# Scores of two of three tiles made three rounds ahead of their selection, in a ring of five rounds

## The chip, the cores and the metric
The kernel runs on 1 core of one Trainium2 chip. The metric is the device time of one execution in microseconds (us); the median over several runs is taken.

## The reference
Three stages in fp32, one behind the other:

```python
# attention: batch 4, 8 heads, 576 tokens, head size 64
scores = scale * np.matmul(q, k.transpose(0, 1, 3, 2))
kth = np.partition(scores, -32, axis=-1)[..., -32:-32 + 1]
scores = np.where(scores >= kth, scores, -1e9)
attn = softmax(scores)                      # exp(s - max) / (sum + 1e-9)
x = matmul(attn, v)                         # -> 2304 x 512
# maxout: d_model 512, d_ff 768
x = np.maximum(np.maximum(x @ w1, x @ w2), x @ w3) @ w_out
# experts: 8, top 1 by x @ w_gate + bias of the row's modality, 512 -> 1024 -> 512
out[mask] = gate_w[mask, None] * (np.maximum(x[mask] @ w1[e], 0.0) @ w2[e])
```

## The kernel before, in words
Attention works in 48 rounds. A round is one block of 192 queries for a pair of heads, 384 rows of scores over 576 keys, held as three tiles of 128 rows: tile 0 and 1 are the first 128 queries of the two heads, tile 2 the remaining 64 of both. Tiles 0 and 1 are folded, which halves what the top-32 selection must search: instead of the scores of each head, TensorE makes the scores against the second half of the keys (index 0, for both heads) and the scores against the difference of the two halves of the keys (index 1, for both heads). From these GpSimd's `fold` makes `upper` and `lower` (the larger and the smaller of each pair of scores) and the scores of the first half. Index 2 is tile 2 in full, against all keys. So only (r, 1) needs `k_diff`, the key differences that GpSimd makes; (r, 0) and (r, 2) go through the same PSUM tile `s_ps`, and (r, 1) through `t_ps` (`d_ps` in the code), which the transposes use too. ScalarE copies (r, 0) and (r, 2) from PSUM to the ring `scores` and (r, 1) to `rise` and `fall` (two instructions).

Each engine runs its own list in order, the rounds being software-pipelined. In round r:

- TensorE (`one_round`, order from `round_items(r)`): the items are Q (a score product), V (the value products of round r-3), H (transposes of the probabilities of round r-2, in five steps) and M (groups of the maxout stage, rounds 6 to 53, and before it W, a product of weights, in rounds 2 to 5). With `AHEAD = 2` the Q items are those of round r+2. The order is Q0, Q1, V, M, H, H, Q2, H, H, M, H, M. The scores of rounds 0 and 1 are made ahead of round 0.
- ScalarE: the copies of these in the same order, and between them the steps of the masked exponential: for round r the scalars, `below` of tiles 0 and 1; for round r-1 `below` of tile 2 (behind Q1) and the three exponentials (behind Q1 to ahead of the copy of Q2).
- VectorE: the selection (MAX8 and MATCH_REPLACE8) of round r, 13 us, and the sums and inverses of round r-1.
- GpSimd, round r: `leave_out(r-1)` (L811, three subtractions of `below`), `add_ways`, `key_differences(r+3)` (L753), `fold(r+2)` (L764, L765, L767), `divide(r-1)` (L819), and up to round 5 `weight_difference(r+2)` (L833).
- SyncE: its queue of loads. In round r it waits for the values' buffer and issues `load_v(r-1)`, then `load_qk(r+4)` (keys L642, queries L643, the rest of the queries in two parts L648) once the tiles of round r+2 are scored, since keys and queries have two slots. Behind the loads of rounds 0 and 1 stand the loads of the weights of the maxout stage, of the biases and of `modality` (one element to a piece).

Maxout takes three groups in a round (`PARTS`), its first group is the first item M of round 6 and waits for all eight weight differences. Up to round 45 there are Q items; then the order is V, M, H, H, M, H, H, M, H. Behind the attention the last rounds finish the maxout stage, and then the experts run.

`scores` has `RING = AHEAD + 2` rounds of three tiles of 576 columns. Counting semaphores carry the order: `scores_ready` (TensorE made a tile) and `scores_copied` (ScalarE copied it) are compared with `scored(r, i)`, the tile's place in the order.

```python
def scored(r, i):
    return r * GROUP + score_order(r).index(i) + 1
```

Of the kernel before, what the change touches and what calls it, by code (L numbers as in the profile page):

```python
# [27 lines left out]
ROUNDS = BLOCKS * RPB  # L28
# [4 lines left out]
GROUP = 3  # L33
REST = BLK - P
AHEAD = 2
LAG = 2
PROB_BUFS = 2
assert PROB_BUFS >= LAG
RING = AHEAD + 2
HALF = SEQ // 2  # L40
FULL = SEQ // P
KB = FULL + 1
# [64 lines left out]
def wait_apart(eng, passed, sem, value):  # L107


    eng.wait_ge(sem, value)  # L110
    eng.sem_inc(passed, 1)
# [65 lines left out]
def score_order(r):  # L177


    return (2, 0, 1) if r == 0 else (0, 1, 2)  # L180


def scored(r, i):


    return r * GROUP + score_order(r).index(i) + 1


def in_range(r):

    return 0 <= r < ROUNDS


def finished_units(r):

    return [(m, g[1]) for m, g in maxout_groups(r) if g[0] == "A" and g[2] == WAYS - 1]
# [5 lines left out]
def round_items(r):  # L202

    ahead, middle, behind = ([("M",) + g for g in groups] for groups in maxout_thirds(r))
    q = [("Q", i) for i in range(GROUP)] if in_range(r + AHEAD) else [None] * GROUP
    h = [("H", c) for c in range(KB)] if in_range(r - LAG) else [None] * KB
    v = ("V",) if in_range(r - LAG - 1) else None
    if in_range(r + AHEAD):  # L210
        items = [q[0], q[1], v] + ahead + h[:2] + [q[2]] + h[2:4] + middle + h[4:] + behind
    else:
        items = [v] + ahead + h[:2] + middle + h[2:4] + behind + h[4:]
    return [item for item in items if item is not None]
# [216 lines left out]
def program(nc, qT, kT, v, w_in, w3T, w_out, w_gate, modality, bias, e_w1, e_w2, shared, x2_dram, list_dram, out):  # L431

    with ExitStack() as ctx:
# [44 lines left out]
        with ExitStack() as held:  # L478
# [10 lines left out]
            v_sb = hb("v_sb", [P, 2, KB, 2 * HEAD])  # L489
            scores = hb("scores", [P, RING, GROUP, SEQ])  # L490
            rise = hb("rise", [P, FOLDED, HALF])
# [53 lines left out]
        passed = sem("passed")  # L545
# [10 lines left out]
        scores_ready = sem("scores_ready")  # L556
        scores_copied = sem("scores_copied")
# [76 lines left out]
        def _(sp):  # L634
            def load_qk(r):

                slot = r % 2
                if r >= 2:

                    sp.wait_ge(scores_ready, (r - 1) * GROUP)  # L640
                k_of = r // (BPB * RPB) * PPB + r % PPB
                sp.dma_start(k_sb[:, slot, :], kT[k_of, :, :]).then_inc(qk_in[slot], 16)  # L642
                sp.dma_start(q_sb[:, slot, :], qT[r, :, 0:P]).then_inc(qk_in[slot], 16)  # L643
                if r < 2:

                    sp.wait_ge(rest_pads_ready, 1)
                for h in range(2):
                    sp.dma_start(q_rest[h * HEAD:(h + 1) * HEAD, slot, h * HEAD:(h + 1) * HEAD],  # L648
                                 qT[r, h * HEAD:(h + 1) * HEAD, P:BLK]).then_inc(qk_in[slot], 16)
# [90 lines left out]
        def _(pool):  # L740
# [15 lines left out]
            def fold(r):  # L756

                slot, ring = r % FOLD_BUFS, r % RING
                wait_apart(pool, passed, scores_copied, scored(r, 1))
# [168 lines left out]
        def _(act):  # L928
# [30 lines left out]
            def copy_scores(r, i):  # L959

                act.wait_ge(scores_ready, scored(r, i))
                part = (d_ps if i == 1 else s_ps)[:, :, 0:HALF]
                if i == 0:
                    nc.scalar.copy(scores[:, r % RING, 0:FOLDED, HALF:SEQ], part).then_inc(scores_copied, 1)
                elif i == 1:
                    if r > 0:

                        act.wait_ge(fold_step, r * 3)
                    nc.scalar.activation(rise[:, :, :], part, ACT.Relu)
                    nc.scalar.activation(fall[:, :, :], part, ACT.Relu, scale=-1.0).then_inc(scores_copied, 1)  # L970
                else:
                    nc.scalar.copy(scores[:, r % RING, i, :].rearrange("p (h n) -> p h n", h=2), part)\
                      .then_inc(scores_copied, 1)
# [52 lines left out]
            def one_round(r):  # L1026
                steps = []
                if in_range(r - 1):
                    steps += [(NEXT_ROUND[name], step) for name, step in zip(STEPS, softmax_steps(r - 1))
                              if name in NEXT_ROUND]  # L1030
                if in_range(r):
                    steps += [(THIS_ROUND[name], step) for name, step in zip(STEPS, softmax_steps(r))
                              if name in THIS_ROUND]
                for m, u in finished_units(r - 1) if r <= LOAD_AT else LAST_UNITS if r == RECTIFY_LAST else []:
                    steps.append((RECTIFY_AT if in_range(r - 1) else -1, lambda m=m, u=u: rectify(m, u)))
                if r == RECTIFY_LAST:
                    for n in range(PIECES // 2):
                        steps.append((-1, lambda n=n: high_piece(0, n)))
                steps.sort(key=lambda step: step[0])
                ran = 0  # L1040
                for item, at in places_in_round(r):

                    while ran < len(steps) and steps[ran][0] < at:
                        steps[ran][1]()
                        ran += 1
                    if item[0] == "H":
                        copy_probsT(r - LAG, item[1])
                    elif item[0] == "Q":
                        copy_scores(r + AHEAD, item[1])
                    elif item[0] == "V":  # L1050
                        copy_out(r - LAG - 1)
                    elif item[2][0] != "Y":
                        copy_moe(*item[1:])
                        if r >= RECTIFY_LAST and item[2] in TURN_AT:
                            for n in TURN_AT[item[2]]:
                                x_high_part(0, n)
                for _, step in steps[ran:]:
                    step()
# [25 lines left out]
            act.wait_ge(sum_pads_ready, 1)  # L1084
            nc.scalar.activation(warm[:, :], sums[:, 0, 0, 1:2], ACT.Exp)
            act.wait_ge(pads_ready, 2)
            for r in range(AHEAD):
                for i in score_order(r):
                    copy_scores(r, i)
            for r in range(LAST_ROUND):  # L1090
                one_round(r)
                if r == COUNT_AT:
# [244 lines left out]
        def _(pe):  # L1337
            def score_tile(r, i):

                slot = r % 2  # L1340
                if i == score_order(r)[0]:
                    pe.wait_ge(qk_in[slot], (r // 2 + 1) * QK_LOADS)
                if i == 1:
                    wait_apart(pe, passed, k_diff_ready, r + 1)
                    turned = (r - AHEAD - LAG) * KB
                    if turned > 0:

                        wait_apart(pe, passed, probsT_copied, turned)
                    elif r > 0:

                        wait_apart(pe, passed, scores_copied, scored(r - 1, 1))
                else:
                    other = scored(r, 2) if (r, i) == (0, 0) else scored(r, 0) if (r, i) != (0, 2) and i == 2 \
                        else scored(r - 1, 2) if r > 1 else scored(0, 0)
                    if (r, i) != (0, 2):

                        wait_apart(pe, passed, scores_copied, other)
                if i < 2:

                    keys = k_sb[:, slot, HALF:SEQ] if i == 0 else k_diff[:, slot, :]  # L1360
                    for h in range(2):
                        ins = nc.tensor.matmul((s_ps if i == 0 else d_ps)[:, h, 0:HALF], q_sb[h * HEAD:(h + 1) * HEAD, slot, :],  # L1362
                                               keys[h * HEAD:(h + 1) * HEAD, :], start=True, stop=True)
                else:

                    for half in range(2):
                        ins = nc.tensor.matmul(s_ps[:, half, 0:HALF], q_rest[:, slot, :],  # L1367
                                               k_sb[:, slot, half * HALF:(half + 1) * HALF], start=True, stop=True)
                ins.then_inc(scores_ready, 1)
# [94 lines left out]
            def one_round(r):  # L1464
                for item in round_items(r):
                    if item[0] == "H":
                        transpose_keys(r - LAG, item[1])
                    elif item[0] == "Q":
                        score_tile(r + AHEAD, item[1])
                    elif item[0] == "V":  # L1470
                        weigh_values(r - LAG - 1)
                    else:
                        moe_group(*item[1:])
# [36 lines left out]
                                               start=(f == 0 and i == 0), stop=(f == FB2 - 1 and i == 2))  # L1510
                ins.then_inc(y_ready, 1)

            for r in range(AHEAD):
                for i in score_order(r):
                    score_tile(r, i)
            for r in range(RECTIFY_LAST):
                one_round(r)
                if r == COUNT_AT:
# [78 lines left out]
```

## Time and profile before

| | us |
|---|---|
| median of 3 runs | 943.24 (943.15 to 943.54) |
| the profiled execution | 943.44 |
| its span, first to last instruction | 941.8 |
| TensorE matmul busy | 897.8 |
| VectorE busy | 720.3 |
| GpSimd busy | 660.1 |
| ScalarE busy | 567.7 |

The profile is of one execution. "Span" is from its first to its last instruction, and what lies around it (1.6 us) is not in the trace. PE is TensorE's matmul, PEld its weight load, DVE is VectorE, ACT is ScalarE, POOL is GpSimd, SP is SyncE. A busy share is an average over stages; the windows give it by stretch.

### The profile page before, as it was taken

The page shows a single profiled execution, that of the slowest core. Times are in us where ns is not written, and L with a number is a line of the kernel's source. Part 1 is how long each engine was busy: PE and PEld are TensorE (multiplying, and loading weights), DVE is VectorE, ACT ScalarE, POOL GpSimd, SP SyncE. Part 2 cuts the span into 40 slices and gives each one's busy share as a digit, 9 for nine tenths or more (in the row PEclk, how much of TensorE's full clock was granted, in tenths as well). Part 3 has the DMA queues.
Part 4 walks back from the last instruction along what each step waited for, and adds up shares of the span by engine and source line. Part 5 has one row for each costly group of instructions (what it writes and reads, how often), then busy time and mean ns, then how long its engine had stood idle before and what let it go on. Part 6 is the DMA issues. An engine that isn't in the chain of part 4 may idle for free.

```text
span 941.8 us, 17739 instructions
## 1 busy us (share of the span) xinstructions
PE 897.8 (95%) x5132; PEld 693.6 (74%) x5133; DVE 720.3 (76%) x2191; ACT 567.7 (60%) x1274; POOL 660.1 (70%) x624
## 2 busy tenths in 40 slices
PE   6688999999999999999999999999999999999997
PEld 2344868668695787759686786858685898998996
DVE  6999999999999999999999999998803721251211
ACT  3577678688877787678786787776533322341221
POOL 7999898988988799878988889885562412231221
PEclk9999999999999999999999999999999999999999
DMA  7721112221211222122121212111052161116110
GB/s 243 220 57 49 53 50 71 82 88 53 66 52 43 70 59 71 43 70 60 46 68 47 82 49 66 47 37 37 14 164 88 40 208 58 54 32 236 45 56 33
DMA packets 69271, 70.84 MB, mean 75 GB/s; under 512 B 15456, under 2 KB 50560, under 8 KB 69184
## 3 DMA queue, kind: packets, MB, share of 16 engines
q1 hardware_dynamic: 65264, 59.44, 20.9%
q0 software_dynamic: 3920, 10.40, 3.5%
q8 instruction: 36, 0.59, 0.2%
q14 instruction: 51, 0.42, 0.1%
HBM read 59.05 MB, written 10.76 MB: 74 GB/s over the span
## 4 chain that ended last, share of the span: by engine, by line
PE 87%; ACT 4%; POOL 3%; issue 3%; DVE 1%; DMA 1%; SPq 1%; POOLq 0%; ACTq 0%; DVEq 0%
PE m_ps L1427 20%; PE m_ps L1509 11%; PE m_ps L1453 9%; PE o_ps L1400 8%; PE s_ps L1492 8%; PE t_ps L1384 7%; PE m_ps L1441 7%; PE s_ps L1367 4%; PE s_ps L1362 3%; PE t_ps L1362 3%; PE o_ps L1492 3%; PE m_ps L1460 2%; POOL scores L811 1%; PE m_ps L1446 1%; DMA q_rest<-queries_t 1%
## 5 line engine op out<-in xcount | busy, mean ns | idle before, releaser
L811 POOL TENSOR_TENSOR scores<-scores,below 128x576 f32<-128x576 f32 x144 | 201.1, 1414 | 65.3 <-ACT below L945 64.7
L1427 PE MATMUL m_ps<-xT,w_sb 128*128 128x192 f32 x1152 | 201.9, 330 | 2.0 <-POOL w_sb L833 2.0
L1427 PEld LDWEIGHTS m_ps<-xT,w_sb 128*128 128x128 f32 x1152 | 187.3, 192 | 5.7 <-issue 5.7
L1155 DVE MAX8 top<-upper 128x8 f32<-128x288 f32 x384 | 159.3, 448 | 0.3 <-issue 0.3
L980 ACT COPY probsT<-t_ps 128x384 f32<-128x384 f32 x240 | 106.6, 491 | 38.2 <-PE t_ps L1384 38.1
L1157 DVE MATCH_REPLACE8 upper<-top,upper 128x288 f32<-128x288 f32 x288 | 125.3, 443 | 0.2 <-issue 0.2
L953 ACT ACTIVATE probs<-scores,shift 128x576 f32<-128x576 f32 x144 | 111.7, 782 | 16.3 <-issue 11.0
L1384 PEld LDWEIGHTS t_ps<-ident,probs 128*128 128x128 f32 x720 | 86.2, 141 | 44.1 <-issue 19.5
L819 POOL TENSOR_SCALAR probs<-probs,inverse 128x576 f32<-128x576 f32 x144 | 105.3, 752 | 16.5 <-DVE inverse L1145 16.5
L1384 PE MATMUL t_ps<-ident,probs 128*128 128x128 f32 x720 | 103.6, 275 | 12.8 <-ACT probsT L980 12.8
L945 ACT ACTIVATE below<-scores,steep_kth 128x576 f32<-128x576 f32 x144 | 109.4, 777 | 2.2
L1155 DVE MAX8 top<-work 128x8 f32<-128x576 f32 x144 | 107.2, 744 | 0.4
L889 POOL DMA_INDIRECT out_rows<-y_sb,info x18 | 17.9, 996 | 108.2 <-ACT y_sb L1081 107.5
L1400 PE MATMUL o_ps<-probsT,v_sb 128*64 128x192 f32 x960 | 88.9, 332 | 2.9 <-issue 2.9
L1453 PE MATMUL m_ps<-wo_sb,stage 128*128 128x512 f32 x192 | 86.3, 598 | 0.0
L1400 PEld LDWEIGHTS o_ps<-probsT,v_sb 128*64 128x64 f32 x960 | 65.7, 137 | 27.4 <-issue 20.8
L1155 DVE MAX8 top<-lower 128x8 f32<-128x288 f32 x192 | 77.2, 445 | 0.0
L1244 DVE SCALAR_TENSOR_TENSOR hTl<-s_ps,hTh 128x384 fp32r<-128x384 f32 x36 | 19.8, 556 | 68.1 <-ACT hTh L1073 68.1
L1157 DVE MATCH_REPLACE8 work<-top,work 128x576 f32<-128x576 f32 x96 | 71.3, 743 | 0.0
L1008 ACT ACTIVATE stage<-m_ps 128x384 f32<-128x384 f32 x72 | 35.1, 488 | 59.3 <-PE m_ps L1427 59.3
L764 POOL TENSOR_TENSOR upper<-scores,rise 128x576 f32<-128x576 f32 x48 | 68.0, 1417 | 0.9 <-ACT fall L970 0.9
L765 POOL TENSOR_TENSOR lower<-scores,fall 128x576 f32<-128x576 f32 x48 | 68.0, 1416 | 0.0
(208 smaller groups left out, 1780.1 us busy)
## 6 DMA issues: line engine op xcount, KB each, us to landing
k_sb<-keys_t SPq DMA_DIRECT2D x48, 288.0 KB, 2.6
v_sb<-values SPq DMA_DIRECT2D x48, 256.0 KB, 2.7
raw<-e_w SPq DMA_DIRECT2D x12, 1024.0 KB, 5.1
maxout_rows<-x_rows SPq DMA_DIRECT2D x18, 256.0 KB, 2.2
q_sb<-queries_t SPq DMA_DIRECT2D x48, 64.0 KB, 2.5
w_sb<-w SPq DMA_DIRECT2D x2, 1536.0 KB, 8.5
q_rest<-queries_t SPq DMA_DIRECT2D x96, 16.0 KB, 2.3
v_sb<-values SPq DMA_DIRECT2D x48, 32.0 KB, 2.6
```

The lines of the kernel that those rows point to most:

```text
L811: nc.gpsimd.tensor_tensor(scores[:, r % RING, i, :], scores[:, r % RING, i, :], below[:, i, :], ALU.subtract).then_inc(masked_ready, 1)
L819: nc.gpsimd.tensor_scalar(part, part, inverse[:, r % 2, i:i + 1], 0.0, ALU.mult, ALU.add)\
L945: nc.scalar.activation(below[:, i, :], scores[:, r % RING, i, :], ACT.Relu, bias=steep_kth[:, top_slot, i:i + 1], scale=-STEEP).then_inc(b ...
L953: nc.scalar.activation(probs[:, r % PROB_BUFS, i, 0:SEQ], scores[:, r % RING, i, :], ACT.Exp, bias=shift[:, top_slot, i:i + 1], scale=SCAL ...
L980: nc.scalar.copy(probsT[:, :, c, :], d_ps[:, c % 2, 0:2 * BLK].rearrange("p (h q) -> p h q", h=2))\
L1155: nc.vector.max(best, src).then_inc(topk_step, 1)
L1157: nc.vector.match_replace(dst, best, src, LOWEST).then_inc(topk_step, 1)
L1384: ins = nc.tensor.transpose(d_ps[:, c % 2, at:at + P], probs[:, r % PROB_BUFS, i, c * P:(c + 1) * P], ident[:, :])
L1400: ins = nc.tensor.matmul(o_ps[h * HEAD:(h + 1) * HEAD, 0:BLK], v_sb[:, slot, c, h * HEAD:(h + 1) * HEAD], probsT[:, h, c, :], start=(c == ...
L1427: ins = nc.tensor.matmul(dst[:, a * BLK:(a + 1) * BLK], w_sb[:, w, c, (first + a) * P:(first + a + 1) * P], xT[:, m % 2, c, b % SPAN * BLK ...
L1453: ins = nc.tensor.matmul(dst[:, :], hT[:, m % 2, j, i * P:(i + 1) * P], wo_sb[:, j, :], start=False, stop=(j == FB - 1))
L1509: ins = nc.tensor.matmul(y_ps[n % 2][:, :], h[:, f, n * P:(n + 1) * P], w[:, f, :], start=(f == 0 and i == 0), stop=(f == FB2 - 1 and i == 2))
```

## The change
`(r, 0)` and `(r, 2)` are made three rounds ahead, in round r-3; `(r, 1)` stays two rounds ahead. The ring has five rounds instead of four. The prologue makes two tiles more, `(2, 0)` and `(2, 2)`. The place of a tile in the order is now looked up in a table, and the load of keys and queries waits for the last tile of the round whose slot it takes.

```diff
-RING = AHEAD + 2
+WHOLE_AHEAD = AHEAD + 1
+RING = WHOLE_AHEAD + 2
...
+def ahead_of(i):
+    return AHEAD if i == 1 else WHOLE_AHEAD
+
+FIRST_SCORES = [(r, i) for r in range(AHEAD) for i in score_order(r)] \
+    + [(r, i) for r in range(AHEAD, WHOLE_AHEAD) for i in (0, 2)]
+SCORES = FIRST_SCORES + [(r + ahead_of(i), i) for r in range(ROUNDS) for i in range(GROUP) if r + ahead_of(i) < ROUNDS]
+SCORED = {tile: n + 1 for n, tile in enumerate(SCORES)}
+DIRECT = [tile for tile in SCORES if tile[1] != 1]
...
 def scored(r, i):
-    return r * GROUP + score_order(r).index(i) + 1
+    return SCORED[r, i]
+
+def all_scored(r):
+    return max(scored(r, i) for i in range(GROUP))
...
-    q = [("Q", i) for i in range(GROUP)] if in_range(r + AHEAD) else [None] * GROUP
+    q = [("Q", i) if in_range(r + ahead_of(i)) else None for i in range(GROUP)]
...
 # load_qk(r), SyncE
-                    sp.wait_ge(scores_ready, (r - 1) * GROUP)
+                    sp.wait_ge(scores_ready, all_scored(r - 2))
...
 # ScalarE, one_round
-                        copy_scores(r + AHEAD, item[1])
+                        copy_scores(r + ahead_of(item[1]), item[1])
...
 # ScalarE, ahead of round 0
-            for r in range(AHEAD):
-                for i in score_order(r):
-                    copy_scores(r, i)
+            for r, i in FIRST_SCORES:
+                copy_scores(r, i)
...
 # TensorE, score_tile(r, i), i = 0 or 2
-                    other = scored(r, 2) if (r, i) == (0, 0) else scored(r, 0) if (r, i) != (0, 2) and i == 2 \
-                        else scored(r - 1, 2) if r > 1 else scored(0, 0)
-                    if (r, i) != (0, 2):
-                        wait_apart(pe, passed, scores_copied, other)
+                    n = DIRECT.index((r, i))
+                    if n > 0:
+                        wait_apart(pe, passed, scores_copied, scored(*DIRECT[n - 1]))
...
 # TensorE, one_round
-                        score_tile(r + AHEAD, item[1])
+                        score_tile(r + ahead_of(item[1]), item[1])
...
 # TensorE, ahead of round 0
-            for r in range(AHEAD):
-                for i in score_order(r):
-                    score_tile(r, i)
+            for r, i in FIRST_SCORES:
+                score_tile(r, i)
```

## Rows read from the trace of the kernel before

**Rows 1.** The page, part 1: busy us, share of the span, instructions.
```profile
PE 897.8 (95%) x5132; PEld 693.6 (74%) x5133; DVE 720.3 (76%) x2191; ACT 567.7 (60%) x1274; POOL 660.1 (70%) x624
```

**Rows 2.** Windows: length, then PE, PEld, DVE, ACT, POOL busy, PEclk, DMA, GB/s.
```profile
26.00:70.00 44.00, 32.67 (x140) 17.92 (x137) 42.71 (x136) 29.62 (x64) 44.00 (x38) 0.96 0.41 124
...
88.00:95.80 7.80, 4.67 (x37) 2.91 (x37) 7.62 (x26) 7.16 (x16) 7.80 (x8) 1.00 0.25 67
...
330.00:440.00 110.00, 108.61 (x671) 81.86 (x670) 106.83 (x339) 83.41 (x197) 96.37 (x87) 1.00 0.21 60
```

**Rows 3.** Timeline at the first maxout group: start, us, engine, line, operation, idle before.
```profile
93.91 1.81 POOL L833 TENSOR_TENSOR w_sb<-w_sb,stage 128x768 f32<-128x768 f32 x1
...
95.86 4.52 PE L1427 MATMUL m_ps<-xT,w_sb 128*128 128x192 f32 x16 [2.01 <-POOL w_sb L833]
```

**Rows 4.** Timeline of a steady round: its score load and the next round's first product.
```profile
385.18 0.33 SPq L642 DMA_DIRECT2D k_sb<-keys_t  x1
...
386.12 1.11 SPq L648 DMA_DIRECT2D q_rest<-queries_t  x2
...
391.27 0.76 PE L1362 MATMUL s_ps<-k_sb,q_sb 64*128 64x288 f32 x4
```

**Rows 5.** The chain that ended last, at the start: start, us, what.
```profile
24.79 1.33 PE s_ps L1362 x4
26.13 0.97 PE t_ps L1362 x4
...
29.81 2.12 DMA q_rest<-queries_t
```

**Rows 6.** Timeline of all engines from 19 to 36 us.
```profile
19.02 0.64 ACT L964 COPY scores<-s_ps 128x576 f32<-128x576 f32 x1 [1.53 <-PE s_ps L1362]
...
20.35 2.29 PE L1367 MATMUL s_ps<-k_sb,q_rest 128*128 128x288 f32 x4
...
22.67 6.11 SPq L642 DMA_DIRECT2D k_sb<-keys_t  x1
...
25.34 1.42 POOL L764 TENSOR_TENSOR upper<-scores,rise 128x576 f32<-128x576 f32 x1
...
29.30 1.11 SPq L648 DMA_DIRECT2D q_rest<-queries_t  x2
...
29.58 0.65 ACT L969 ACTIVATE rise<-t_ps 128x576 f32<-128x576 f32 x1 [2.68 <-POOL scores L767]
...
30.66 0.78 ACT L945 ACTIVATE below<-scores,steep_kth 128x576 f32<-128x576 f32 x1
...
31.21 4.12 POOL L811 TENSOR_TENSOR scores<-scores,below 128x576 f32<-128x576 f32 x3
...
35.28 0.80 POOL L753 TENSOR_TENSOR k_diff<-k_sb 128x288 f32<-128x288 f32 x1
```

**Rows 7.** DMA issues from 14 to 40 us: count, KB each, us to landing.
```profile
mod<-modality SPq DMA_DIRECT2D x1, 18.0 KB, 9.0
```

**Rows 8.** The chain that ended last, round 45: (47, 0), then (47, 2).
```profile
624.08 0.69 PE s_ps L1362 x4
...
631.56 0.97 PE s_ps L1367 x4
```

**Rows 9.** Timeline: pairs of probability copies and the transposes behind them, two places.
```profile
88.28 0.86 ACT L980 COPY probsT<-t_ps 128x384 f32<-128x384 f32 x2
...
88.81 0.93 PE L1384 MATMUL t_ps<-ident,probs 128*128 128x128 f32 x6 [0.89 <-ACT probsT L980]
...
631.42 0.87 ACT L980 COPY probsT<-t_ps 128x384 f32<-128x384 f32 x2
...
632.37 0.82 PE L1384 MATMUL t_ps<-ident,probs 128*128 128x128 f32 x6
```

**Rows 10.** Timeline of VectorE in round 46.
```profile
649.85 0.16 DVE L1140 TENSOR_REDUCE full_sum<-sums 128x3 f32<-128x6 f32 x1 [2.13 <-ACT probs L953]
```

**Rows 11.** TensorE's waits from 90 to 640 us: us in total, times, longest.
```profile
PE t_ps L1384 <- ACT probsT L980: 6.5, 7, 1.1
```

More of the change, by code:

```diff
@@ L180, in score_order @@
     return (2, 0, 1) if r == 0 else (0, 1, 2)
+def ahead_of(i):
[4 more added lines that the diff above has]
+SCORED = {tile: n + 1 for n, tile in enumerate(SCORES)}
+assert len(SCORED) == len(SCORES) == ROUNDS * GROUP
+DIRECT = [tile for tile in SCORES if tile[1] != 1]
 def scored(r, i):
-    return r * GROUP + score_order(r).index(i) + 1
+    return SCORED[r, i]
+def all_scored(r):
+    return max(scored(r, i) for i in range(GROUP))
 def in_range(r):
```

## Prediction
> **How I read it.** The windows come first, to see which engine has no slack in which stretch; then what ends the wait at the seam between two stretches; then the timeline around the moved tiles, at the start and at the end. A tile is written (round, index): the change moves (r, 0) and (r, 2), not (r, 1).
>
> **What bounds the kernel now.** TensorE is busy for 897.8 of 941.8 us, GpSimd for 660.1 [rows 1]. By stretch it is two machines. From 26 to 70 us GpSimd is busy for all of its 44.00 us, TensorE for 32.67; from 88 to 95.8 GpSimd for 7.80 of 7.80, TensorE for 4.67. From 330 to 440 us TensorE is busy for 108.61 of 110, GpSimd for 96.37 [rows 2]. The seam is at 95.86: the first maxout group has kept TensorE idle for 2.01 us, until GpSimd's last weight difference, begun at 93.91, was done [rows 3]. Before the seam a wait of GpSimd costs its full length, since it has no idle time to make it up from; behind the seam only TensorE's work and idle time count.
>
> **What stays.** Every product, copy and fold is still made once. In rounds 3 to 44 the items stand in the same places, and each product into the shared score bank still waits for the copy before it. The ring grows with the distance, so its reuse adds no wait. Steady rounds should keep their length if keys and queries come in time. These have to be there a round earlier: tile (r+4, 0) opens round r+1, no longer r+2. Take one steady round: its score load goes out from 385.18 to 386.12 + 1.11 = 387.23; 2.12 us later, at 389.4, it has landed, and the next round opens at 391.27 [rows 4, 5]. Even sent as late as now it is in time, and it may go earlier, since it waits for (r+2, 1) and no longer for (r+2, 2). SyncE's other loads of the round are in front of it as before. Cost: nothing, under the cover of these 1.9 us and more; without it a round loses what is missing.
>
> **The start, where two tiles are added.** The prologue gets (2, 0) and (2, 2), which were round 0's; round 0 then makes (3, 0), (2, 1), (3, 2), and round 1 opens with (4, 0). TensorE has room for all of it. But (2, 1) and (3, 1) stand behind more than before, and GpSimd waits for their copies.
> Step 1. (2, 0) is copied at 19.02 for 0.64 us, as now. Then (2, 2), 2.29 long at this clock [rows 6], runs from 19.8 to 22.1; its copy ends near 22.8; (3, 0) starts then and (2, 1) ends 1.33 + 0.97 = 2.30 later [rows 5], at 25.1. Its two copies are over 1.2 us on (from 29.58 to just behind 30.66 in the round shown), at 26.4. The fold of round 2 starts at 25.34 now: it is 1.1 us late. A weight difference of 1.81 and two of the three subtractions (L811, 4.12 for three) are queued behind it; the third is reached at about 35.1, where it now starts at about 33.9 [rows 3, 6].
> Step 2. This third subtraction needs ScalarE's third `below` of round 0, which stands behind the copies of (3, 1). On TensorE (3, 1) stands behind (4, 0) after the change, and (4, 0) needs the load of round 4. SyncE begins that load at 22.67 and is held in it for 6.11 us, its last part goes out at 29.30, and the chain has it landed at 29.81 + 2.12 = 31.93 [rows 5, 6]. After the change SyncE comes to it at 25.1, when (2, 1) is scored, which is inside the hold. I take the hold to have a fixed end, because the load of the modality, of 18 KB in tiny pieces and issued just before, takes 9.0 us to land [rows 7], about as long as the hold lasts. So 31.93 stays; the same load sent later can't well land earlier.
> Step 3. (4, 0) starts at 31.97, (3, 1) ends 2.30 later at 34.3, its first copy starts at 34.4, `below` 1.08 after that (29.58 to 30.66 now) at 35.45, and ends 0.78 later at 36.25. The third subtraction starts about 0.15 behind it and takes 1.4: it ends at 37.8. The key difference behind it starts at 35.28 now [rows 6]. That is 2.5 us lost, and the 1.1 of step 1 are inside them. VectorE's sum for round 0 needs the last exponential, which stands behind the same subtraction, so VectorE is late by the same and no more.
> Step 4. Does anything swallow it? Behind it on GpSimd are fold 3, a division, and in order everything up to the weight difference of rows 3, with no idle time between, so the seam moves from 95.86 to 98.4. Is more added? (5, 0) waits for the copy of (4, 2), which stands behind the last exponential: 37.8 + 0.8 + 0.7 = 39.4. (4, 1) ends 2.3 later near 41.8, and its copy can't begin before fold 3 ends at 37.8 + 0.8 + 4.2 = 42.8. Nothing is added.
>
> The price of the hold can be doubted from a page. The Trainium skill (DMA: Bandwidth & Descriptors, section "Anatomy of one DMA — SWDGE (gpsimd) path") calls descriptor generation a small part of a transfer's fixed cost, of which many can be emitted before it shows; it speaks of another issuing path than SyncE's. The row of 6.11 us says otherwise for this load; by the page alone it would land before 29 us after the change too, only step 1 would be lost, and the sum would be 943.3. I keep the row.
>
> **The end, where two tiles are gone.** Round 45 has only (47, 1) left. On the chain there (47, 0) has 0.69 us and (47, 2) 0.97 [rows 8]. Without the first, the value products start right behind (47, 1), and 0.69 is gained. The second covers a copy as well. The transposes behind it need the pair of copies that begins at 631.42. Where a pair begun at 88.28 had no cover, the next six transposes started at 88.81 and ended at 89.74, 1.46 behind the copies' start; here that makes 632.88, against 632.37 + 0.82 = 633.19 now [rows 9]. So 0.3 of the 0.97 comes through. Sum 1.0; bounds nothing (both only covered) and 1.66 (neither did). VectorE doesn't take it back: in the next round it waits for ScalarE for 2.13 us [rows 10]. All behind is released by TensorE and moves along.
>
> **Sum.** +2.5 - 1.0 = +1.5 us. The profiled execution took 943.44 with a span of 941.8 and would take 944.9; it lies 0.2 over the median, so on 943.24 it makes 944.7. Bounds of the start: 1.1 if the load is never waited for, 5.0 if the hold keeps its length. The small steps may be off by 0.6 together, so the likeliest case alone spans 944.0 to 945.3.
>
> **Rivals.**
> A. The hold is a duration and not an end. SyncE is free at 25.1 + 6.1 = 31.2, the load lands at 34.4, 2.5 later, and the start costs 5.0: 943.24 + 5.0 - 1.0 = 947.2, slower. For it: there is only this one hold to judge by. Against: the slow load in front of it. It decides once the load lands 0.4 us later than now, as each us over 31.93 goes straight to the seam and 945.13 is the bound below. Chance 0.15.
> B. The load is earlier, and only step 1 is lost: 943.3. It needs a landing before 29.3, which a later issue can hardly give. Chance 0.09.
> C. GpSimd's delay is swallowed before the seam and only the end counts: 942.2. Against: 7.80 busy of 7.80. Chance 0.07.
> D. The larger distance frees the steady rounds: the waits of the transposes for ScalarE's copies, 7 of them with 6.5 us in all between 90 and 640 us [rows 11], go away: 943.24 + 1.5 - 6.5 = 938.2. Against: the score copy in front of it keeps its place. Chance 0.04.
> E. In steady rounds the score load comes late after all; a quarter of a us in each of 40 rounds is 10 us, 955. Against: rows 4. Chance 0.03.
> The forecast as worked out has 0.62.
>
> **Numbers.** A measurement of this kernel tells a change of about 0.2% from none, that is 1.9 us: same is 941.35 to 945.13. Slower: A, E and, as 944.7 lies near the bound, 0.12 of the forecast's 0.62, together 0.30. Faster: D and a little of C, 0.05. Same: 0.65. The range leaves out C, D, E and the outer parts of A and B, in all under 0.2: 943.0 to 947.3.
>
> **What would show it.** In the profile after: the hold of the `k_sb` load ending near 28.8 again; a GpSimd wait of about 1.1 us before the fold of round 2 and of about 1.3 before the third L811 of round 0; (4, 0) at 32.0; the first maxout group near 98.4, with some 2 us idle before it; still 6.5 us in waits for copies in the steady rounds; round 45 shorter by about 1.0. I am wrong if the hold ends past 29, if GpSimd shows idle time between 40 and 95 us, or if steady rounds change their length.

## The result and the profile after
The changed kernel took 944.13 us (median of 20 runs, 942.65 to 946.22), the kernel before 941.97 in the same comparison (20 runs, 941.6 to 943.69). The ratio is 1.0017, with a 95% interval of 1.0011 to 1.0023: 1.6 us more, on 943.24 some 944.8 (the two medians lie 2.2 us apart, at the upper end of the interval). Forecast were 944.7 and 0.16% more. The size is right, but the profile shows that two terms of the sum were too large and almost offset each other. The 943.24 of three runs, on which the forecast was built, lies in the upper of two groups of the kernel before: of its 20 runs 13 took 941.6 to 942.17 and 7 took 943.15 to 943.69.

The timeline of the changed kernel at the start and at the seam (line numbers are its own: L662 is the load of keys, L784 the fold, L831 the subtraction, L1380 and L1445 the score product and the maxout group):
```profile
25.12 1.85 SPq L662 DMA_DIRECT2D k_sb<-keys_t  x1
...
26.50 1.41 POOL L784 TENSOR_TENSOR upper<-scores,rise 128x576 f32<-128x576 f32 x1 [1.20 <-ACT fall L990]
...
30.56 1.33 PE L1380 MATMUL s_ps<-k_sb,q_sb 64*128 64x288 f32 x4 [3.45 <-DMA q_rest<-queries_t]
...
32.35 4.15 POOL L831 TENSOR_TENSOR scores<-scores,below 128x576 f32<-128x576 f32 x3
...
33.96 0.78 ACT L965 ACTIVATE below<-scores,steep_kth 128x576 f32<-128x576 f32 x1
...
36.44 0.81 POOL L773 TENSOR_TENSOR k_diff<-k_sb 128x288 f32<-128x288 f32 x1
...
97.02 2.84 PE L1445 MATMUL m_ps<-xT,w_sb 128*128 128x192 f32 x16 [2.00 <-POOL w_sb L853]
```
They answer to [rows 6] and [rows 3]. The fold of round 2 starts at 26.50 after a wait of 1.20 us, where 1.1 was expected. But SyncE's hold (the time for which it is kept in one issue, here that of the keys of round 4) ends at 26.97, not at 28.78; (4, 0) starts at 30.56, the third `below` ends at 34.74, and GpSimd, which comes to the third subtraction only at about 35.1, finds it ready. The key difference is at 36.44 against 35.28, the first maxout group at 97.02 against 95.86: 1.16 us, and none of the second wait. TensorE idles 2.00 us ahead of the seam as before.

The waits of TensorE from 90 to 640 us (total, times, longest) and a window of the steady rounds, from one wait for a copy to another, first after the change and then before it:
```profile
PE t_ps L1402 <- ACT probsT L1000: 7.8, 9, 1.1
...
PE t_ps L1380 <- ACT probsT L1000: 0.7, 1, 0.7
```
```profile
126.40:580.50 454.10, 447.33 (x2733) 333.17 (x2733) 441.65 (x1402) 346.29 (x812) 400.44 (x361) 1.00 0.22 63
...
126.90:580.80 453.90, 447.20 (x2733) 333.28 (x2733) 441.33 (x1401) 346.41 (x812) 400.49 (x361) 1.00 0.21 62
```
The steady rounds kept their length within 0.2 us: 454.10 against 453.90, and the bounds are rounded. From the wait at 144.01 to the one at 580.80 it is 436.79 us before the change; after it, from 143.69 to 580.55, it is 436.86. The waits for copies are 7.8 us in 9 where [rows 11] had 6.5 in 7; one of the nine, 0.90 at 89.98, was moved into the window by the delay ([rows 9] show it at 88.81), and one of 0.40 in round 45 is new. The other seven are those of [rows 11]. The second row, 0.7 us, is new. The chain shows where it stands:
```profile
623.49 0.34 PE t_ps L1402 x3
623.84 0.02 issue
623.86 0.49 ACT probsT L1000
624.35 0.14 issue
624.48 0.76 PE t_ps L1380 x4
625.24 1.78 PE o_ps L1418 x20
...
631.16 0.50 ACT probsT L1000
631.66 0.04 issue
631.70 0.93 PE t_ps L1402 x6
632.63 5.15 PE m_ps L1471 x12
...
638.89 1.85 PE o_ps L1418 x20
```
This is round 45 [rows 8]. (47, 0) is gone, but (47, 1), which uses the PSUM tile of the transposes, now waits 0.65 us for the copy of the last ones. That copy was covered by (47, 0). From the last transposes of round 44 to the value products of round 46 it is 638.89 - 623.49 = 15.40 us; in the kernel before 639.44 - 623.75 = 15.69. The end gives 0.3, not 1.0. All ten profiles of this document agree on it: 15.69 in the three of the kernel before and its variants, 15.39 or 15.40 in the six in which (47, 2) is gone from round 45, and 15.68 in the one in which only (47, 0) is.

The spans of the two profiled executions can't be compared as they are (941.3 after, 941.8 before). The first maxout group took 2.84 us in this profile and 4.52 in [rows 3], for the same 16 products. Here the granted clock had been full (2.4 GHz) since 43.85, there it fell to half (1.2 GHz) for 3.4 us as the group began, after the same 2 us without work. So the part behind the seam says little until profiles with the same clock are put beside each other. The seam is the start of the first maxout group; from it to the value products of round 46 it is, in us (index 0 alone is left out, since TensorE waits for loads there):

| kernel | clock falls at the seam | clock stays full |
|---|---|---|
| before, and its two variants | 543.58, 543.60, 543.61 | no profile |
| with (47, 2) gone from round 45 | 543.31 in all three | 541.82, 541.87, 541.90 |

At the same clock the two kernels differ behind the seam, up to there, by the 0.3 of the end and nothing else. The fall costs 1.4 to 1.5 us. With 1.16 for the start, 0.3 for the end and 1.45 for the clock the profile after should be 0.6 us shorter than the one before, and it is: 942.85 against 943.44. All three profiles of the kernel before show the fall; that its lower group of runs is that without it fits the 1.4 us between the groups, but no profile shows it.

### The profile page after: what moved, and what is told of

Same layout as the page of the kernel before. It is cut to its first block, busy times and chain, and to the rows that moved or that the text cites. A ratio compares the mean times of both kernels' runs of the same rounds, so it can differ in the third digit from the quotient of the medians.

```text
span 941.3 us, 17739 instructions
## 1 busy us (share of the span) xinstructions
PE 897.5 (95%) x5132; PEld 692.0 (74%) x5133; DVE 720.0 (76%) x2191; ACT 567.7 (60%) x1274; POOL 659.1 (70%) x624
## 4 chain that ended last, share of the span: by engine, by line
PE 83%; issue 5%; DVE 4%; ACT 3%; POOL 2%; DMA 1%; SPq 1%; DVEq 0%; POOLq 0%; ACTq 0%
PE m_ps L1445 19%; PE m_ps L1527 11%; PE m_ps L1471 9%; PE o_ps L1418 8%; PE s_ps L1510 8%; PE t_ps L1402 6%; PE m_ps L1459 6%; PE s_ps L1385 4%; PE s_ps L1380 3%; PE o_ps L1510 3%; PE t_ps L1380 3%; DVE top L1174 2%; PE m_ps L1478 2%; DMA q_rest<-queries_t 1%; PE m_ps L1464 1%
## 5 line engine op out<-in xcount | busy, mean ns | idle before, releaser
L831 POOL TENSOR_TENSOR scores<-scores,below 128x576 f32<-128x576 f32 x144 | 201.5, 1421 | 63.4 <-ACT below L965 62.9
L1445 PE MATMUL m_ps<-xT,w_sb 128*128 128x192 f32 x1152 | 200.3, 328 | 2.0 <-POOL w_sb L853 2.0
L1445 PEld LDWEIGHTS m_ps<-xT,w_sb 128*128 128x128 f32 x1152 | 185.6, 190 | 5.7 <-issue 5.7
L784 POOL TENSOR_TENSOR upper<-scores,rise 128x576 f32<-128x576 f32 x48 | 68.2, 1422 | 2.1 <-ACT fall L990 2.1
L1028 ACT ACTIVATE stage<-m_ps 128x384 f32<-128x384 f32 x72 | 35.1, 488 | 57.0 <-PE m_ps L1445 57.0
```

What stands on the lines that cost most here:

```text
L831: nc.gpsimd.tensor_tensor(scores[:, r % RING, i, :], scores[:, r % RING, i, :], below[:, i, :], ALU.subtract).then_inc(masked_ready, 1)
L1445: ins = nc.tensor.matmul(dst[:, a * BLK:(a + 1) * BLK], w_sb[:, w, c, (first + a) * P:(first + a + 1) * P], xT[:, m % 2, c, b % SPAN * BLK ...
```

## The experiments
All times are against the kernel before on the same chip. On the chips of the experiments it took 950.8 and 951.2 us (the last section says where), and its runs spread over 4.5 and 5.1 us, so a time alone tells 1 us from nothing badly. The profiles, read at the seam (95.86 in [rows 3]) and in round 45, tell 0.1 to 0.2. The views around the seam often end within the first maxout group, so that the length shown there is that of a part; its start is what counts.

**The key-difference tile first in rounds 0 and 1.**
```diff
-SCORES = ... for i in range(GROUP) ...
+SCORES = ... for i in ((1, 0, 2) if r < 2 else (0, 1, 2)) ...
-        items = [q[0], q[1], v] + ahead + ...
+        items = (q[1::-1] if r < 2 else q[:2]) + [v] + ahead + ...
-    first = {"Q0": 0, "Q1": 1, ...
+    first = {"Q0": 5 if r < 2 else 0, "Q1": 1, ...
```


> The changed kernel with one difference: in rounds 0 and 1 the tile (r+2, 1) is made and copied ahead of (r+3, 0), and (4, 0) behind the exponentials of round 1. All else, the ring and the end too, is as in the change. My theory: the loss is made by the fold and the third subtraction of GpSimd waiting for (2, 1) and (3, 1) at the start. Then no wait of GpSimd is left between 16 and 96 us, the first maxout group starts near 95.9, the loss of 1.2 us or more is gone, and the end's gain of 0.3 stays: 0.3 us under the kernel before (0 to 0.6). Rival 1, the loss lies in the steady rounds or in the larger ring: about 1.6 us over the kernel before, as the change. Rival 2, the loss is the end's and not the start's: also over it by 1 or more.


Measured: ratio 1.0001 (0.9991 to 1.001). Its timeline at the fold of round 2, the third subtraction and the seam:
```profile
25.22 1.42 POOL L786 TENSOR_TENSOR upper<-scores,rise 128x576 f32<-128x576 f32 x1
...
31.07 4.15 POOL L833 TENSOR_TENSOR scores<-scores,below 128x576 f32<-128x576 f32 x3
...
35.16 0.81 POOL L775 TENSOR_TENSOR k_diff<-k_sb 128x288 f32<-128x288 f32 x1
...
95.85 1.62 PE L1447 MATMUL m_ps<-xT,w_sb 128*128 128x192 f32 x7 [2.02 <-POOL w_sb L855]
```
No wait is shown at the fold, and the seam is at 95.85. The ring of five, the steady rounds and the end are those of the change, so the start is where it loses, and the order of the tiles there is the reason. The interval of its time (0.9 less to 1.0 more) holds the forecast 0.3 less and leaves out the rival's 1.6 more. From its wait for a copy at 144.00 to the one at 580.82 it is 436.82 us, where the kernel before has 436.79.

**Each index alone.** `ahead_of` gives three for one index only, and the prologue gets that tile alone:
```diff
-    return AHEAD if i == 1 else WHOLE_AHEAD
+    return WHOLE_AHEAD if i == 2 else AHEAD      # or i == 0
```


> One part alone: only (r, 2) is made three rounds ahead, (r, 0) stays at two; the ring has five rounds. My theory: (2, 1) is then copied ahead of the time at which GpSimd reaches its fold, and (3, 1) stands behind no late load, so the start costs nothing (maxout starts near 95.9), and (47, 2) gone from round 45 gains 0.3: 0.3 us under the kernel before (0 to 0.6). The rival, that each tile moved into the prologue pushes GpSimd back: 0.5 to 1 over it.

> The other part alone: only (r, 0) is made three rounds ahead. My theory: no wait before the fold of round 2, but (3, 1) stands behind (4, 0) and so behind the load of round 4; if that lands between 30.4 and 31.9 us, the third subtraction of round 0 is late by 1.0 to 2.5 us, and the seam with it. The end gains nothing, since (47, 1) then waits for the last copy where (47, 0) stood. So 1.0 to 2.5 us over the kernel before, as much as the whole change. Rival (the clock of TensorE at the seam makes the difference): no more than 0.3 over it.


Measured: index 2 alone 0.9996 (0.9983 to 1.0008), which by the time alone holds the forecast and its rival; the seam decides for the forecast:
```profile
95.72 1.54 PE L1445 MATMUL m_ps<-xT,w_sb 128*128 128x192 f32 x8 [2.02 <-POOL w_sb L853]
```
Index 0 alone took 1.0078 (1.0052 to 1.0104), 7.4 us more, far beyond the forecast. The waits of TensorE with index 0 alone, from 14 to 640 us, and one steady round of it:
```profile
PE s_ps L1380 <- DMA q_rest<-queries_t: 24.7, 11, 6.4
```
```profile
256.08 0.33 SPq L662 DMA_DIRECT2D k_sb<-keys_t  x1
...
256.93 1.11 SPq L668 DMA_DIRECT2D q_rest<-queries_t  x2
...
259.63 0.76 PE L1380 MATMUL s_ps<-k_sb,q_sb 64*128 64x288 f32 x4 [0.80 <-DMA q_rest<-queries_t]
```
With index 2 still two rounds ahead, the score load can't be released before (r+2, 2), late in the round, while (r+4, 0) opens the next: TensorE waits for the load, 11 times. Six of these waits lie ahead of the seam (one of them, at (2, 0), every kernel has), and the seam is at 101.99, 6.1 late; five are in the steady rounds, 0.80 to 0.93 us each and some 110 us apart, 4.3 in all. That is rival E in part, which the change itself escapes, by this reading because there the load waits for (r+2, 1): from 90 to 640 us it shows no wait for a load. My sentence "Even sent as late as now it is in time" was right for the round I took it from and wrong as a statement on all rounds. The profile has (4, 0) at 30.91 and a wait of 1.06 us of GpSimd in front of the third subtraction, as step 2 has it, and a second one of 2.67 at 89.67, in front of a later third subtraction; the rest of what this run loses is TensorE's own waiting for loads.
At the end the two parts divide as said: from the last transposes of round 44 to the value products of round 46 it is 648.27 - 632.59 = 15.68 with index 0 alone (nothing gained) and 639.03 - 623.64 = 15.39 with index 2 alone (all of the 0.3). Rows of the chain, index 0 alone:
```profile
632.59 0.34 PE t_ps L1402 x3
632.93 0.02 issue
632.95 0.49 ACT probsT L1000
633.44 0.14 issue
633.57 0.76 PE t_ps L1380 x4
```

**The modality load out of the way.** In the changed kernel it moves behind the weights of round 1.
```diff
-            sp.dma_start(mod64[:, :], modality...).then_inc(ids_in, 16)
 ...
                     load_weights(wg_sb[:, :, :], w_gate, w3_in_sem)
+                    sp.dma_start(mod64[:, :], modality...).then_inc(ids_in, 16)
```


> The changed kernel with the load of the modality (18 KB in pieces of one element) moved behind the weights in SyncE's queue of round 1, out of the way of the load of round 4. My theory: the hold of 2 to 6 us in that load goes, it lands before 29.3 us, and of the start's loss only the wait of 1.2 us before the fold of round 2 stays: 0.9 us over the kernel before, and runs closer together than the change's 3.6 us from lowest to highest. The rival, that the runs spread by the clock of TensorE at the seam: the same spread and the same 1.6 us as the change.


Measured: 1.0008 (0.9997 to 1.0018), 0.8 us more, an interval that holds the rival's 1.6 as well; 2.65 us from lowest to highest in 12 runs.
```profile
25.85 0.34 SPq L662 DMA_DIRECT2D k_sb<-keys_t  x1
...
27.23 1.40 POOL L784 TENSOR_TENSOR upper<-scores,rise 128x576 f32<-128x576 f32 x1 [1.27 <-ACT fall L990]
...
29.57 0.76 PE L1380 MATMUL s_ps<-k_sb,q_sb 64*128 64x288 f32 x4 [1.53 <-DMA q_rest<-queries_t]
```
The hold is gone (0.34 us), and the load that is issued next behind the modality in its new place, that of round 6 at 41.13, is held for 1.79. So it is the modality load that makes the hold. The wait of 1.27 before the fold stays, and the seam is at 97.72; 0.57 of these 1.86 us come from GpSimd's later start in this execution. That the runs lie closer is not shown: twelve runs beside twenty are few.

Where the hold ends can be read from the three other runs on this chip, the key-difference tile first, index 2 alone and index 0 alone:
```profile
22.76 4.75 SPq L664 DMA_DIRECT2D k_sb<-keys_t  x1
```
```profile
21.91 5.66 SPq L662 DMA_DIRECT2D k_sb<-keys_t  x1
```
```profile
24.58 2.93 SPq L662 DMA_DIRECT2D k_sb<-keys_t  x1
```
SyncE comes to the load at three times 2.7 us apart, and is let go at 27.51, 27.57 and 27.51. In all ten profiles the hold ends 0.8 to 1.0 us ahead of the landing of the modality load. That landing took 8.9 to 9.7 us from its issue in nine of them and 7.4 in the first profile of the changed kernel; why it was short there isn't known. In nine of the ten the load of 1536 KB in front of it lands within 0.2 us of the end of the hold too, but in the run of this section the hold of 1.79 ends 3.1 us behind the landing of such a load and still 0.9 ahead of the modality's.

**The changed kernel again, and a GpSimd operation more.** The second adds, to the kernel before, in front of the fold of round 2:
```diff
+                if r == 2:
+                    nc.gpsimd.tensor_tensor(spare[:, :, :], second, rise[:, :, :], ALU.add)
```


> The changed kernel unaltered, to have a second profile of it and its time beside the next three. Forecast of the theory (the start costs the larger of 1.2 us and what the load of round 4 lands behind 29.3 us, the end gives 0.3): 0.9 to 2 us over the kernel before. First maxout group 1.2 us or more later than 95.86 counted from the same start of (2, 0); round 45 to 46 at 0.3 less behind the last wait of the transposes than in the kernel before.

> The kernel before with one more GpSimd operation of 1.4 us (a sum into a spare tile) in front of the fold of round 2; the result is unused. If GpSimd sets the time up to the seam, as rows 2 and 3 say, the first maxout group starts 1.4 later and the kernel takes 1.4 us more. The rival, that the 2 us that TensorE waits at the seam are set by a chain beside GpSimd (copies, loads) as well, so that a small delay is swallowed: 0 to 0.5.


Measured: 1.0017 (1.0004 to 1.0031) and 1.0002 (0.9992 to 1.0013). The changed kernel's second profile differs from its first in the hold:
```profile
25.24 2.93 SPq L662 DMA_DIRECT2D k_sb<-keys_t  x1
...
26.62 1.40 POOL L784 TENSOR_TENSOR upper<-scores,rise 128x576 f32<-128x576 f32 x1 [1.29 <-ACT fall L990]
...
31.50 1.33 PE L1380 MATMUL s_ps<-k_sb,q_sb 64*128 64x288 f32 x4 [4.58 <-DMA q_rest<-queries_t]
...
35.86 1.40 POOL L831 TENSOR_TENSOR scores<-scores,below 128x576 f32<-128x576 f32 x1 [0.62 <-ACT below L965]
...
97.90 2.53 PE L1445 MATMUL m_ps<-xT,w_sb 128*128 128x192 f32 x7 [2.02 <-POOL w_sb L853]
```
Here (4, 0) starts 0.94 us later, and the second wait of step 2 is there, 0.62 us. The seam is at 97.90, 2.04 later than in the kernel before, with 0.09 of that from a later (2, 0). So the two profiles put the start's price at 1.2 and 1.9 us, and with the 0.3 of the end the change costs 0.9 and 1.6.
With one GpSimd operation more, in the kernel before:
```profile
25.16 1.43 POOL L766 TENSOR_TENSOR spare<-scores,rise 128x576 f32<-128x576 f32 x1
...
97.13 3.38 PE L1430 MATMUL m_ps<-xT,w_sb 128*128 128x192 f32 x10 [2.01 <-POOL w_sb L836]
```
The seam is at 97.13, 1.27 late, in an execution in which GpSimd was 0.2 us sooner ahead of the fold. GpSimd's time does reach the seam, and it is all still there at the value products of round 46 (640.73 against 639.44). The time of the whole kernel is another matter: 0.2 us more with an interval of -0.8 to 1.2, which just leaves out the forecast of 1.4 and holds the rival's 0 to 0.5. That is a miss of the forecast. The profile shows no place up to 640 us where the delay is swallowed, and what lies behind (the wait of the last section is 2 us longer in this one profile) can't be told apart from scatter. So the claim that a delay of GpSimd costs the kernel its full length rests on the profiles up to 640 us and on the next run.

**The load of round 4 later, in both kernels.** The load of w_out (1536 KB) moves in front of it.
```diff
+            load_weights(wo_sb[:, :, :], w_out, w3o_in_sem)
             for r in range(LAST_ROUND):
 ...
-                if r == 0:
-                    load_weights(wo_sb[:, :, :], w_out, w3o_in_sem)
```


> The changed kernel with the load of w_out (1536 KB) put in front of the load of round 4 in SyncE's queue instead of behind it, so that this lands some 3 to 5 us later, near 35. My theory of the start: (4, 0) and with it (3, 1) wait for it, the third subtraction of GpSimd ends about 5.9 us behind the landing, and the seam moves by 3 to 6 us more than in the change: 4 to 7 us over the kernel before. Rival, that (3, 1) behind (4, 0) doesn't matter and only the wait before the fold of round 2 counts: as the change, 1 to 2.

> The control: the kernel before with the same reordering of the two loads. There (4, 0) opens round 2 and is made at 36.94, so a landing up to about 36 costs nothing: 0 to 0.5 us over the kernel before. If the load order costs time by another way, this shows it and is to be taken off the run before it.


Measured: the changed kernel 1.0053 (1.0034 to 1.0072), 5.0 us; the kernel before 1.0021 (1.0006 to 1.0036), 2.0 us. First the changed kernel, then the kernel before:
```profile
34.94 1.33 PE L1379 MATMUL s_ps<-k_sb,q_sb 64*128 64x288 f32 x4 [8.06 <-DMA q_rest<-queries_t]
...
39.29 1.40 POOL L830 TENSOR_TENSOR scores<-scores,below 128x576 f32<-128x576 f32 x1 [4.61 <-PE s_ps L1384]
```
```profile
36.59 0.79 POOL L752 TENSOR_TENSOR k_diff<-k_sb 128x288 f32<-128x288 f32 x1 [1.23 <-DMA q_rest<-queries_t]
...
36.97 1.33 PE L1361 MATMUL s_ps<-k_sb,q_sb 64*128 64x288 f32 x4 [7.66 <-ACT scores L971]
...
97.25 3.18 PE L1426 MATMUL m_ps<-xT,w_sb 128*128 128x192 f32 x10 [2.02 <-POOL w_sb L832]
```
(4, 0) starts at 34.94 and the third subtraction ends at 40.69, 5.75 behind it, the delay of step 3 (5.8). GpSimd waits 0.66 before the fold and 4.61 here, and the seam moved to 101.22, by 5.4. The profile puts this wait down to a score product; I take it to be `below` behind (3, 1), since the subtraction starts 0.17 us behind its end, as in the second profile of the changed kernel, and 4.35 behind the start of (4, 0), where it was 4.36 in that profile and with index 0 alone. In the control my "a landing up to about 36 costs nothing" missed a wait: GpSimd's key difference of round 4 needs the load too, waits 1.23 for it, and the seam moved by 1.39. The same reordering moved the seam of the changed kernel from 97.02 or 97.90 to 101.22, by 3.3 to 4.2, so 1.9 to 2.8 more than that of the kernel before. The times say the same with less precision: 5.0 us over the kernel before, 2.0 in the control. The rival (as the change, 1 to 2) is out, the 5.0 have an interval of 3.2 to 6.8.

**What GpSimd lost and where the seam went.** GpSimd's start is read at its key difference at 18.00 in the kernel before, and the seam at 95.86.

| profile | GpSimd's start | lost by GpSimd up to the seam | seam |
|---|---|---|---|
| changed kernel | -0.09 | 1.20 | +1.16 |
| changed kernel again | -0.08 | 1.29 + 0.62 | +2.04 |
| modality load out of the way | +0.57 | 1.27 | +1.86 |
| key-difference tile first | -0.13 | 0 | -0.01 |
| index 2 alone | -0.22 | 0 | -0.14 |
| before, GpSimd operation more | -0.19 | 1.43 | +1.27 |
| changed, load of round 4 later | 0.00 | 0.66 + 4.61 | +5.36 |
| before, load of round 4 later | 0.00 | 1.23 | +1.39 |

In all eight the seam moves by the sum of the two columns in front of it, within 0.2 us.

## Why the prediction came out right
- **What bounds the kernel** held: what GpSimd lost before 96 us was found at the seam within 0.2 us in eight profiles (the table above), with TensorE's 2.0 us of idle time ahead of it. Only with index 0 alone did late loads hold TensorE itself there. The steady rounds kept their length.
- **Step 1** held: 1.20 and 1.29 us of wait before the fold, 1.1 expected; gone when (r, 1) goes first.
- **Step 2** had the right mechanism and a term mis-sized: "I take the hold to have a fixed end" was right in kind: the end hangs on the modality load and not on when SyncE comes (27.51, 27.57, 27.51 above). But that load does not land at the same time in each execution, and the end moves with it: 28.78 in the profile before, 26.97 and 28.17 in those after, 28.11 in the kernel before with the GpSimd operation. So "the same load sent later can't well land earlier" was false: (4, 0) started at 30.56 and 31.50 and not at 31.97. These 31.97 are the term that was too large.
- **Step 3**: so the second wait was 0 and 0.62 us where 1.3 was predicted, the start's price 1.2 and 1.9 where it was 2.5. Rival B (only step 1) is what the first profile shows and a piece of step 2 what the second does; rival A is refuted, by the holds of 1.85 and 2.93 us. B's condition, a landing before 29.3, was too strict: by the sum itself, 2.5 lost at a landing at 31.93 of which 1.1 are step 1, the load adds nothing up to 30.5. In the first profile (4, 0) started at 30.56 and added nothing. So B's chance of 0.09 was too low for a reason that the prediction's own numbers held.
- **The end** failed in the 0.69 of (47, 0). I had looked at what the value products wait for and not at (47, 1) itself, which waits for the copy of the transposes that stand in its PSUM tile. It gave nothing (15.68 against 15.69, index 0 alone). The 0.3 of (47, 2) was as computed.
- The errors, 0.6 to 1.3 us too much loss at the start and 0.7 too much gain at the end, offset each other. That the forecast of 1.5 came within 0.1 of the measured 1.6 is luck; that the change loses some 1 to 2 us at the start, by the path of steps 1 to 3, and gains a little at the end is what the prediction had right. The 944.7 itself lies 0.6 over the measured median of 944.13, since it was built on the upper group of the kernel before.
- Rivals C and D didn't occur. E is real, in five steady rounds, for a kernel that moves index 0 alone.

## What to carry to other kernels
A tile moved ahead of the loop is paid for not by its own time but by what stands behind it in order on each engine. Ask which engine has no idle time in that stretch, and whether the product that it waits for has fallen behind one with a load in front of it. The same tiles in another order cost nothing here. And an instruction that is taken away at a round's start or middle gives back its time less the copy it covered; look for the wait of the very next instruction, not of the one after it.

## What the runs showed of the hardware
- A load of 18 KB in pieces of one element held SyncE in the next load it issued, for 1.79 to 6.11 us where that was the load of keys and for 7.57 and 8.27 where it was that of w_out; with it elsewhere the same issue took 0.34 us. The hold ended 0.8 to 1.0 us ahead of the landing of the 18 KB, in all ten profiles.
- The first maxout group takes 2.84 us at the full granted clock and 4.52 where the clock falls to its lower level (half) as it begins, after the same 2.0 us without work; 1.4 to 1.5 us of it are left at the end of the attention. Both cases occurred with the changed kernel.
- On the chips of the experiments both kernels took some 9 us more than in the first comparison (950.8 and 951.2 against 941.97, and 953.1 against 944.1). With the key-difference tile first, ScalarE stood still for 6.0 us behind the last value products, and TensorE from 689 us with it; the row of its wait names no instruction of the trace:
```profile
ACT xT L1009 <- remote: 6.0, 1, 6.0
...
PE m_ps L1447 <- ACT xT L1009: 2.4, 1, 2.4
```
  What it waited for wasn't found. It is 6.0 to 6.1 us in seven of the eight profiles taken there and 8.1 in the one with the added GpSimd operation, and the first comparison's two profiles have none at that place. With the key-difference tile first the stretch from 685 to 730 us is 45.0 long, and its counterpart in the kernel before 37.7. So this shifts all kernels of the experiments nearly alike; its scatter lies in the times of whole kernels, and that is one more reason to read the profiles at the seam and in round 45, both ahead of it.
